# Sums of squares split into two single-rate products, two weight loads ahead of a store, and sums of weights made earlier, in a fused attention and double-MLP kernel

## What is computed

```python
def _moe_ref(x, w_gate, w_val, w_out, rms_g):
    rms = np.sqrt(np.mean(x * x, axis=-1, keepdims=True) + 1e-06)
    xn = x / rms * rms_g
    g = xn @ w_gate
    silu = g * (1.0 / (1.0 + np.exp(-g)))
    val = xn @ w_val
    return (silu * val @ w_out)

def _moe2_ref(x, w_in, w_out):
    h = x @ w_in
    g = h * (1.0 / (1.0 + np.exp(-1.702 * h)))
    return (g @ w_out)

def reference(**kwargs):
    attn_out = _attn_ref(...)          # batch 4, 8 heads, 576 tokens, head size 64, window 64
    x = attn_out as [2304 tokens, 512]
    x = _moe_ref(x, ...)               # 512 -> 1536 -> 512
    return _moe2_ref(x, ...)           # 512 -> 2048 -> 512
```

## Time and profile before

| | before |
|---|---|
| median of 3 runs (lowest to highest) | 910.84 us (910.81 to 911.53) |
| time of the profiled execution | 911.02 us |
| its span in the trace | 909.2 us |
| mean granted clock of PE | 0.996 |
| PE busy | 894.0 us, 98% of the span |
| PE weight loads (beside its matmuls) | 772.9 us, 85% |
| DVE busy | 537.1 us, 59% |
| ACT busy | 396.2 us, 44% |
| POOL busy | 81.7 us, 9% |

### The profile page before, as it was taken

One profiled execution on the slowest core, in us unless ns is written; L12 is line 12 of the kernel. 1 busy time (PEld: TensorE's weight loads), 2 busy tenths in 40 slices (PEclk: granted clock), 3 DMA queues, 4 the chain that ended last, 5 costly groups with the idle time before them and its releaser, 6 DMA issues.

```text
span 909.2 us, 14697 instructions
## 1 busy us (share of the span) xinstructions
PE 894.0 (98%) x5372; PEld 772.9 (85%) x5372; DVE 537.1 (59%) x1251; ACT 396.2 (44%) x937; POOL 81.7 (9%) x114
## 2 busy tenths in 40 slices
PE   8799999999999999999999999999999999999998
PEld 7799888888888888888888888899989999899997
DVE  6886533334433343333336467887788787867663
ACT  5666333343333433334113444545455454544442
POOL 6234001130011200112000000000000000000000
PEclk9999999999999999999999999999999999999999
DMA  7672111102112011101400232121432122141201
GB/s 253 205 215 93 50 50 51 52 22 73 50 50 74 14 60 50 53 22 41 145 1 24 70 116 70 47 93 47 163 116 80 60 70 70 51 159 47 70 24 70
DMA packets 41079, 69.77 MB, mean 77 GB/s; under 512 B 3632, under 2 KB 13872, under 8 KB 41008
## 3 DMA queue, kind: packets, MB, share of 16 engines
q1 hardware_dynamic: 39600, 67.12, 22.7%
q10 hardware_dynamic: 1408, 1.70, 0.5%
HBM read 59.38 MB, written 9.44 MB: 76 GB/s over the span
## 4 chain that ended last, share of the span: by engine, by line
PE 92%; DVE 4%; ACT 2%; issue 1%; DMA 1%; SPq 0%; ACTq 0%
PE ps L618 16%; PE ps L619 15%; PE ps L620 15%; PE ps L812 7%; PE ps L813 7%; PE ps L811 7%; PE ps L750 6%; PE ps L754 6%; PE ps L752 6%; PE ps L603 2%; PE ps L575 2%; PE ps L589 2%; DVE w_all L1178 1%; DMA wstage<-in_w_b 1%; ACT prob L854 0%
## 5 line engine op out<-in xcount | busy, mean ns | idle before, releaser
L618 PE MATMUL ps<-x_hi,w_all 128*128 128x512 f32 (+1 forms) x480 | 181.2, 377 | 0.2 <-DVE x_lo L1118 0.2
L620 PE MATMUL ps<-x_lo,w_all 128*128 128x512 f32 (+1 forms) x480 | 176.9, 369 | 0.0
L619 PE MATMUL ps<-x_hi,w_all 128*128 128x512 f32 (+1 forms) x480 | 176.9, 369 | 0.0
L812 PE MATMUL ps<-w2out,hB 128*128 128x512 f32 x288 | 113.4, 394 | 0.0
L813 PE MATMUL ps<-w2out,hB 128*128 128x512 f32 x288 | 113.4, 394 | 0.0
L811 PE MATMUL ps<-w2out,hB 128*128 128x512 f32 x288 | 112.6, 391 | 0.0
L618 PEld LDWEIGHTS ps<-x_hi,w_all 128*128 128x128 f32 x480 | 90.5, 188 | 19.3 <-issue 3.9
L619 PEld LDWEIGHTS ps<-x_hi,w_all 128*128 128x128 f32 x480 | 90.5, 189 | 15.3 <-issue 1.0
L620 PEld LDWEIGHTS ps<-x_lo,w_all 128*128 128x128 f32 x480 | 90.5, 189 | 15.2
L1216 DVE SCALAR_TENSOR_TENSOR sig<-sig,ps 128x512 f32<-128x512 f32 x48 | 33.0, 686 | 108.5 <-ACT sig L964 108.5
L618 PE MATMUL ps<-h_hi,w_all 128*128 128x512 f32 (+1 forms) x240 | 90.0, 375 | 1.7 <-DVE hid L1225 1.5
(11 more groups left out here) (137 smaller groups left out, 1551.6 us busy)
## 6 DMA issues: line engine op xcount, KB each, us to landing
wstage<-in_w_b SPq DMA_DIRECT2D x48, 512.0 KB, 3.5
wstage<-in_w_a SPq DMA_DIRECT2D x36, 256.0 KB, 3.3
vwin<-in_v_win SPq DMA_DIRECT2D x32, 256.0 KB, 3.7
kwin<-in_k_t SPq DMA_DIRECT2D x32, 160.0 KB, 3.3
x2raw<-x_scratch SPq DMA_DIRECT2D x3, 1536.0 KB, 7.9
out_dram<-yB SPq DMA_DIRECT2D x18, 256.0 KB, 4.3
qtok<-in_q_t SPq DMA_DIRECT2D x34, 128.0 KB, 2.5
x_scratch<-wstage SPq DMA_DIRECT2D x3, 1024.0 KB, 4.2
```

Of the source, the lines that this page charges most:

```text
L618: pe.matmul(out_, w[:, 0, cols], xh, start=first, stop=False, **flags)
L619: pe.matmul(out_, w[:, 1, cols], xh, start=False, stop=False, **flags)
L620: return pe.matmul(out_, w[:, 0, cols], xl, start=False, stop=last, **flags)
L812: pe.matmul(y, h[:, rows], w[:, 1, chunk, :], start=False, stop=False)
```

## The change

Three edits. **(1)** For the tiles 1 to 4 the float32 matmul of `sum_squares` is replaced by two `fp32r` matmuls, of a high part `ss_hi` (copied by ACT, `sum_hi`, between `tanh_A` and `hid_hi_A` of chunk 10) and a low part `ss_lo` (subtracted by DVE between `hidden_A` and `hid_lo_A` of chunk 10), against `ones_r`, a copy of `ones` that DVE makes once, in chunk 10 of tile 0. The new tiles lie where `probT` lies. The sum for tile 0 stays as it was. **(2)** On SP, unit 4 (w_out(1)) is loaded ahead of `load_x2(1)` and unit 5 (w_in(3)) ahead of `store_x2(4)`. **(3)** In the pairs 0, 8 and 16 `combine_w2(g + 2)` stands ahead of `make_c(g, C22)` and no longer at the pair's end.

```diff
-            probT = sb("probT", [P, 2, GB * P], F32, at)
+            with ExitStack() as pt:
+                probT = sb("probT", [P, 2, GB * P], F32, pt)
+            ss_hi = sb("ss_hi", [P, TMAX], F32R, at)
+            ss_lo = sb("ss_lo", [P, TMAX], F32R, at)
+            ones_r = sb("ones_r", [P, P], F32R, at)
...
             load_w2(in_unit(2))
+            load_w2(out_unit(1))
             load_x2(1)
+            load_w2(in_unit(3))
             store_x2(NA - 1)
             for g in range(1, NP):
-                load_w2(out_unit(g))
-                if g + 2 < NP:
+                if g > 1:
+                    load_w2(out_unit(g))
+                if 1 < g < NP - 2:
                     load_w2(in_unit(g + 2))
...
                 if t == 0:
                     pe.wait_ge(early_sums, EARLY - 1)
                     pe.wait_ge(probT_ready, EARLY - 1)
-                else:
-                    pe.wait_ge(squares_done, SQ * (steps_of(t)[1] // PAIRS - 1))
-                pe.matmul(ps[:, ATT_BANK, 0:n], ones[:, :], ss[:, 0:n], start=True, stop=True).then_inc(sumsq_done, 1)
+                    pe.matmul(ps[:, ATT_BANK, 0:n], ones[:, :], ss[:, 0:n], start=True,
+                              stop=True).then_inc(sumsq_done, 1)
+                    return
+                pe.wait_ge(ss_split, t)
+                pe.matmul(ps[:, ATT_BANK, 0:n], ones_r[:, :], ss_hi[:, 0:n], start=True, stop=False)
+                pe.matmul(ps[:, ATT_BANK, 0:n], ones_r[:, :], ss_lo[:, 0:n], start=False,
+                          stop=True).then_inc(sumsq_done, 1)
...
+            def sum_hi(t):
+                act.wait_ge(squares_done, SQ * (steps_of(t)[1] // PAIRS - 1))
+                nc.scalar.copy(ss_hi[:, :], ss[:, :]).then_inc(ss_hi_made, 1)
+
...
                     tanh_A(t, c)
+                    if c == SUMSQ_AT and t + 1 < NA:
+                        sum_hi(t + 1)
...
                     hidden_A(t, c)
+                    if t == 0 and c == CA - 2:
+                        dve.wait_ge(ones_ready, 1)
+                        nc.vector.tensor_copy(ones_r[:, :], ones[:, :])
+                    if c == SUMSQ_AT and t + 1 < NA:
+                        dve.wait_ge(ss_hi_made, t + 1)
+                        nc.vector.tensor_tensor(ss_lo[:, :], ss[:, :], ss_hi[:, :].bitcast(F32),
+                                                ALU.subtract).then_inc(ss_split, 1)
...
                     w2out_lo(g, 1)
+                if p == 0:
+                    combine_w2(g + 2)
                 if p > 0 and j + 1 < NB:
...
-                if g + 2 < NP:
+                if p > 0 and g + 2 < NP:
                     combine_w2(g + 2)
                 hid_lo_B(g, C12)
```

More of the change, by code:

```diff
@@ L206, in fused_attention_mlps @@
         squares_done = sem("squares_done")
+        ss_hi_made = sem("ss_hi_made")
+        ss_split = sem("ss_split")
         sumsq_done = sem("sumsq_done")
```

## The result

| | before | after |
|---|---|---|
| median (lowest to highest), 4 runs each | 911.18 us (910.81 to 912.1) | 903.9 us (903.13 to 904.1) |
| profiled execution, its span | 911.02, 909.2 us | 904.1, 901.6 us |

A forecast was written before the change was run, and what follows sets the result against it. PE, busy 98% of the span, bounds the kernel. Pairs -6.3, sums in tiles 1 to 3 -1.2, tile 0 +0.6 make -6.9: 911.0 to 904.1, less 0.2 for the median, 903.9 us; own range 903.4 to 904.5, 8 in 10 902.9 to 905.6.

The forecast's parts named there:

- Pair 1: First MLP pair after pair 0: with edits (2) and (3) it loses its whole excess over pair 2, 5.38 us.
- needs this edit too: Pair 1's first wait comes from the sums of weights, so edit (3) is needed there besides edit (2).
- Pairs 9 and 17: Pairs behind first pairs 8 and 16: edit (3) removes their excess, 2 x 0.47 = 0.94 us.
- The sums in tiles 1 to 3: Two fp32r matmuls replace the float32 one on PE: 0.41 us saved in each tile, 1.2 us together.
- Tile 0: The new cast delays ACT's chain in chunks 10 and 11, for which PE waits: costs 0.6 us.
- 1.3 as an upper bound: Tile 0's cost if cast and subtraction should add up (0.62 + 0.69).
- Pair 1 kept no second bound: Rival: DVE's splits in pair 1 end behind product_5, PE waits for C22; about 1 us stays, 904.9; chance 8%.
- the sums got cheaper: Rival: the sums in tiles 1 to 3 do not get cheaper; 1.2 us are missing, 905.1; chance 7%.
- tile 0 was not free: Rival: tile 0 costs nothing, as the idle 1.08 us take the cast; 903.3; chance 8%.
- The clock did not fall in tile 0: Rival: waits at tile 0's end bring the clock down; 1.7 us on top, 905.6; chance 10%.
- The late weights of pair 8: Rival: combine_w2 waits for unit 19 and holds make_c; landing after 22 us gives 914.8 us or so; chance 1%.

The follow-up runs named there:

- loads_only: Edit (2) alone on the kernel before: 906.79 us against 910.85, ratio 0.9958; pair 1 lasts 16.64 us.
- wsums_only: Edit (3) alone on the kernel before: 910.59 us against 910.85, ratio 0.9996; pair 1 lasts 20.77 us.
- sums_only: Edit (1) alone on the kernel before: 908.97 us against 910.85, ratio 0.9981.
- act_tables2: The changed kernel with two more table loads on ACT ahead of the cast of the high part in tile 0: 907.01 us.
- act_tables1: The changed kernel with one more table load on ACT ahead of the cast in tile 0: 905.47 to 906.26 us in three executions, a fourth (2278 us) left aside.
- dve_shift5: The kernel before with the mask's one memset split into six, five more DVE instructions: 910.47 against 911.28 us, ratio 0.9993.

## Why the prediction was right, point by point

**Pair 1.** Right in size and in mechanism: 5.38 us, all of it, since pair 1 has the work and the order of pair 2. The two edits are not two shares, though. loads_only takes 4.31 us and wsums_only 0.18 at most; the missing 0.9 come only with both. The prediction said that pair 1 "needs this edit too"; the experiments put numbers on it. It gave the whole of edit (2) as one term; only unit 4 mattered.

**Pairs 9 and 17.** Right: 0.90 of 0.94 us, with the idle time left ahead of C22 as worked out. Pair 17 was taken as pair 9 over again, but had 0.44 us to lose and not 0.47.

**The sums in tiles 1 to 3.** Right in mechanism; 1.34 us came where 1.2 stood. The stretch at the sum itself gives 0.42 us each, 1.26; the rest lies in the steps right behind it: from 188.78 to the matmul at 192.18 it took 3.40 us before, the same stretch 2.95 after (189.11 to 192.06), so 0.45 us a tile.

**Tile 0.** Right that it costs, and that ACT's chain is what costs: 0.47 us against 0.6. The term was sized by the cast's record of 0.62 us, but what counts is the step to the next instruction, 0.53, as two casts in a row overlap by 0.09 us; and Ln had stood 0.08 us behind the end of its table load before and stands 0.02 behind it now, which leaves 0.47. Where the prediction let cast and subtraction add up to 1.3 as an upper bound, the stretch in the changed kernel and in sums_only (0.48) excludes it.

**What it did not have.** Pair 4's 0.30 us. A pair length of 15.87 us was in the trace of before, one row away from those that I used; I had compared pair 1 with pairs 2 and 3 and pair 9 with pair 2, and not looked at the others. The gain there belongs to no edit's purpose.

**The rivals.** Pair 1 kept no second bound, the sums got cheaper, tile 0 was not free. The clock did not fall in tile 0. Behind a longer wait, 3.10 us, it does; the price I gave it, 1.7 us, was twice what it cost there. That price rests on 1.7 us of lost clock in 4 us; the words beside it, that half of these 4 us ran at 1.2 GHz, are wrong, as 1.7 us lost at half speed are 3.4 us. The rule of the Trainium skill that stood beside this rival (TensorE: Matmul & The Clock Gate, "What's actually happening"), that activity is what releases the throttle, agrees with both traces: in act_tables2 the clock came back to 1.00 while PE worked on without a wait. That sentence alone does not tell whether a particular wait will bring the clock down: 1.81 us did not here, 1.96 us in pair 1 did, in company with two shorter ones. The late weights of pair 8 were not provoked, and so that rival's price was not tried; by its own working (each microsecond beyond 655.8 paid twice) weights that take 22 us to land would give about 915.9 us, not 914.8.

**The total.** Of the 0.7 us by which the stretches beat my sum, 0.30 are pair 4, 0.14 the sums, 0.13 tile 0 and 0.16 the start, less 0.04 for pairs 9 and 17. That the median still is 903.9 is partly chance: I subtracted 0.2 us for the median against the profiled execution, and the traced execution after the change has a short span, 901.6 us, where the two in the middle of the four have 902.0 and 902.1. By the stretches alone it would have been 910.8 - 7.6 = 903.2.

## What to carry to other kernels

When a loop's passes hold the same work, compare the lengths of all of them, each one: the excess holds waits, slow clock and late issues at once, and bounds what an edit can give. A transfer that waits in its queue behind a store is as late as the store's producer; look for what stands ahead of the late issue before touching the engine that waits. Two fixes of one stall are not worth the sum of their parts: one alone can merely move the wait, and only the fix of the wait that ends last pays.

## What the runs showed of the hardware

- A clock drop costs less than its own loss where PE would wait next: 3.4 us at 1.2 GHz (about 87.5 to 90.9 us in act_tables2) cost 0.83 us in a stretch with later waits, against about 1.7 us in pair 1 before the change.
- At the same place of the program, a wait of 1.81 us followed by steady work left the granted clock at 1.00 (act_tables1), one of 3.10 us did not (act_tables2); one trace of each.
- Two table loads in a row take 2.57 us, 1.28 each, and the next cast starts right behind them.
- Moving DVE's instructions by five places, at 1 us, let one instruction near 587 us start 0.36 us earlier in its pair, and took 0.30 us off that pair (dve_shift5); whole executions don't show it, and the cause is open.
